# Routed half slots: the next rows' transposes go between the two parts of layer 1's transposes, and layer 2 multiplies high parts before low parts

## The reference, cut to what matters

```python
logits = x @ w_gate
noise_scale = np.log1p(np.exp(x @ w_noise))
noisy_logits = logits + noise_scale * noise
top2 = np.argpartition(-noisy_logits, 2, axis=1)[:, :2]
...
for e in range(E):
    for k in range(2):
        mask = top2[:, k] == e
        h = np.maximum(x[mask] @ w1[e], 0.0)
        out[mask] += top2_w[mask, k, None] * (h @ w2[e])
```

## Time and profile before

| | |
|---|---|
| median of 3 runs | 1065.53 us (1064.56 to 1066.09) |
| profiled execution, time | 1066.34 us |
| profiled execution, span first to last instruction | 1064.6 us |
| TensorE matmul, busy | 1001.9 us, 94% of the span |
| TensorE weight load, busy | 930.5 us, 87% |
| VectorE, busy | 748.9 us, 70% |
| ScalarE, busy | 475.4 us, 45% |
| GpSimd, busy | 165.6 us, 16% |
| mean granted TensorE clock | 0.964 of full speed |

### The profile page before, as it was taken

How to read it: one execution, slowest core, us unless ns; L and a number is a source line. 1 busy time by engine, 2 the same in 40 slices (tenths; PEclk the granted TensorE clock), 3 DMA queues, 4 the chain that set the end, 5 groups by cost and what they waited for, 6 DMA issues and landing times.

```text
span 1064.6 us, 25662 instructions
## 1 busy us (share of the span) xinstructions
PE 1001.9 (94%) x10317; PEld 930.5 (87%) x10317; DVE 748.9 (70%) x1812; ACT 475.4 (45%) x707; POOL 165.6 (16%) x164
## 2 busy tenths in 40 slices
PE   4777989999999999999999999999999999999995
PEld 4675878789889888889899999999999999999994
DVE  6989497389489488542548876767767786776774
ACT  4511423523532622422245554556465564654563
POOL 0000000021012012022305321122121112112111
PEclk7579899899999999999999999999999999999998
DMA  9160031042042033024575544335162425536221
GB/s 324 45 152 1 4 104 36 22 131 52 22 122 63 3 88 76 3 70 155 179 244 179 121 120 120 86 50 171 23 179 45 148 53 154 166 52 169 39 38 23
DMA packets 71459, 102.03 MB, mean 96 GB/s; under 512 B 28624, under 2 KB 59856, under 8 KB 70992
## 3 DMA queue, kind: packets, MB, share of 16 engines
q1 hardware_dynamic: 59296, 78.51, 24.4%
q0 software_dynamic: 10992, 20.70, 10.2%
q10 hardware_dynamic: 1088, 1.65, 0.5%
HBM read 140.53 MB, written 29.51 MB: 160 GB/s over the span
## 4 chain that ended last, share of the span: by engine, by line
PE 83%; DVE 7%; ACT 3%; issue 2%; SPq 2%; DMA 1%; DVEq 0%; POOLq 0%; ACTq 0%
PE ps L1595 39%; PE ps L1741 21%; PE ps L1636 7%; PE ps L1478 3%; PE ps L1572 2%; PE ps L1562 2%; PE ps L1552 2%; PE ps L1461 2%; PE ps L1652 1%; PE ps L1513 1%; PE ps L1523 1%; DVE prod L977 1%; DVE x L981 1%; DVE joint L1015 1%; PE ps L1534 1%
## 5 line engine op out<-in xcount | busy, mean ns | idle before, releaser
L1595 PE MATMUL ps<-xr,wr_in 128*128 128x512 f32 x972 | 240.0, 400 | 3.4 <-DVE xr L1045 1.9
L1741 PE MATMUL ps<-w2r,hbT 128*128 128x384 f32 x1320 | 237.0, 337 | 0.8 <-DVE hbT L1265 0.3
L1741 PEld LDWEIGHTS ps<-w2r,hbT 128*128 128x128 f32 x1320 | 227.9, 188 | 2.5 <-DVE hbT L1265 2.5
L1595 PEld LDWEIGHTS ps<-xr,wr_in 128*128 128x128 f32 x972 | 180.9, 190 | 44.3 <-DVE xr L1045 2.3
L1595 PE MATMUL ps<-xbT,w1r 128*128 128x256 f32 x1728 | 211.0, 283 | 0.0
L1595 PEld LDWEIGHTS ps<-xbT,w1r 128*128 128x128 f32 x1728 | 210.1, 192 | 0.0
L639 POOL DMA_INDIRECT out_rows<-yb,idx x55 | 91.1, 1656 | 380.0 <-DVE yb L1277 291.3
L1091 DVE TENSOR_TENSOR w1r<-w1s,w1r 128x768 fp32r<-128x768 f32 x128 | 121.2, 957 | 19.3 <-ACT w1r L776 17.1
L792 ACT ACTIVATE hbT<-ps 128x512 fp32r<-128x512 f32 x96 | 57.3, 597 | 170.5 <-PE ps L1595 169.0
L776 ACT CAST w1r<-w1s 128x768 fp32r<-128x768 f32 x128 | 104.4, 828 | 24.9 <-DMA w1s<-in_we 24.9
L1091 DVE TENSOR_TENSOR w2r<-w2s,w2r 128x768 fp32r<-128x768 f32 x128 | 113.8, 951 | 1.4 <-ACT w2r L780 1.4
(11 more groups left out here) (209 smaller groups left out, 1019.3 us busy)
## 6 DMA issues: line engine op xcount, KB each, us to landing
w1s<-in_we SPq DMA_DIRECT2D x32, 1536.0 KB
w2s<-in_we SPq DMA_DIRECT2D x32, 1536.0 KB
xb<-rows SPq DMA_DIRECT2D x25, 402.0 KB
kv_s<-in_kv SPq DMA_DIRECT2D x24, 384.0 KB, 3.3
k_s<-in_k SPq DMA_DIRECT2D x12, 512.0 KB, 3.6
joint<-in_q SPq DMA_DIRECT2D x24, 256.0 KB
out_rows<-padrow SPq DMA_DIRECT2D x13, 384.0 KB, 4.4
w_in<-in_w_blocks SPq DMA_DIRECT2D x3, 1152.0 KB, 10.6
```

Source lines behind the costliest of these rows:

```text
L1595: mm = pe.matmul(dst, w, m, start=(n == 0), stop=(n == len(todo) - 1))
L1741: mm = pe.matmul(ps[:, 6 + h, 0:MD], hbT[:, a, f, h * P:h * P + P], w2r[par][:, b, f], start=(f == 0 and n == 0), stop=(f == FT2 - 1 and n ...
```

## The change

In a half slot, `block_rows(j + 1)` is issued between `half_h(group, 0)` and `half_h(group, 1)` and no longer behind both. Layer 2 of a half slot becomes a function of its own: for each group of four f, first the eight matmuls with the high part of h, which wait for ScalarE's cast (`s_gh`), then the four with the low part, which wait for VectorE's subtraction (`s_g`). The matmuls are the same 24. There are four waits in place of two. Full slots keep their order.

```diff
-            def expert_out(j, par, half):
+            def expert_out(j, par):
-                for h in range(1 if half else 2):
+                for h in range(2):
...
-                        if half and f % 4 == 0:
-                            pe.wait_ge(s_g, j * 4 + (f // 2 + 2))
-                        elif not half and h == 0 and f % 2 == 0:
+                        if h == 0 and f % 2 == 0:
                             pe.wait_ge(s_g, j * 4 + (f // 2 + 1))
...
-                    mm.then_inc(p_yb, 2 if half else 1)
+                    mm.then_inc(p_yb, 1)
+
+            def half_expert_out(j, par):
+
+                for g in range(2):
+                    for a, low_parts in ((0, (0, 1)), (1, (0,))):
+                        pe.wait_ge(s_g if a else s_gh, j * 4 + (2 * g + 2))
+                        for f in range(4 * g, 4 * g + 4):
+                            for b in low_parts:
+                                mm = pe.matmul(ps[:, 6, 0:MD], hbT[:, a, f, 0:P], w2r[par][:, b, f],
+                                               start=(f == 0 and a == 0 and b == 0), stop=(f == FT2 - 1 and a == 1))
+                mm.then_inc(p_yb, 2)
...
                     half_h(group, 0)
+                    block_rows(j + 1, 1 - par, next_half)
                     half_h(group, 1)
...
-                block_rows(j + 1, 1 - par, next_half)
+                if not half:
+                    block_rows(j + 1, 1 - par, next_half)
...
-                expert_out(j, par, half)
+                if half:
+                    half_expert_out(j, par)
+                else:
+                    expert_out(j, par)
```

## The result

| | before | after |
|---|---|---|
| median of 12 runs each | 1065.81 us | 1062.60 us |
| range | 1063.70 to 1071.06 | 1060.48 to 1064.00 |
| profiled execution, time | 1066.34 us | 1063.64 us |
| span | 1064.6 us | 1061.9 us |
| mean granted TensorE clock | 0.964 | 0.964 |

The ratio is 0.9971 with a 95% interval of 0.9959 to 0.9982, so the change is faster by 0.29%. The forecast median was 1062.6 us.

A forecast was written before the change was run, and what follows sets the result against it. PE nearly always busy, VectorE's xbT chain limiting the gain: five slots of 0.71 - d - 0.05, one of 0.98 - d - 0.05, minus d at the end; with d = 0.19, 2.9 us off 1065.53 gives 1062.6 us, range 1061.0 to 1064.8.

The forecast's parts named there:

- The two waits and their size: Half slots: weight loads idle seven times for second hb (3.4 us) and for hbT's first low part (2.5 us).
- The six transposes fill the first wait; d = 0.19: Half slot: moved transposes fill the hb wait but delay the second four, and ScalarE's second cast, by d, 0.19 us.
- High parts first: Layer 2 of a half slot: loads start at 983.34 against 984.15, a head start of 0.81 us.
- Two more waits cost nothing: Layer 2 of a half slot: four waits in place of two, already satisfied, cost zero.
- What is late next: Next slot's first load: xbT late, a new wait of about 0.35 us, six times; gain 0.47 us, not 0.81.
- The end: Last half slot: TensorE's head start is worth nothing, the output's scaling comes the full delay, 0.19 us, later.
- The sum: Whole kernel: 4.23 - 7d over five slots, slot 6 and the end; 2.9 us gained with d = 0.19.
- A: Rival: VectorE's chain does not limit the next slot; about 4.7 us gained, 1060.8 us; chance 0.05.
- B: Rival: larger delay of the second transposes, 0.30 to 0.60 us; gain 2.1 to 0, say 1064.5 us; chance 0.24.
- C: Rival: late rows or slow transposes delay the second transposes; with d = 1.0, 2.8 us slower, 1068.3 us; chance 0.03.
- D: Rival: fourteen transposes in a row drop the clock to 1.2 GHz for layer 2; 22.6 us, 1088; chance 0.01.
- E: Rival: nothing changes, the gaps are the model's and the real array never idled; 1065.5 us; chance 0.04.

The follow-up runs named there:

- e5: The change, with quarter 2 of the next w1 put between the two hbT parts on ScalarE and VectorE; 1055.46 us, ratio 0.9961 to before.
- e3: The change, with the next rows' six transposes between the two parts issued twice; 1062.47 us, ratio 1.0020 to before.
- e1: Kernel before, with only the next rows' transposes moved between the two parts, layer 2 in old order; 1059.73 us, ratio 1.0000 to before.
- e2: Kernel before, with only layer 2's high parts first, the next rows' transposes still behind both parts; 1057.75 us, ratio 0.9976 to before.

## Why the prediction was right

**The two waits and their size.** Right: both are gone, 0.84 us in each half slot.

**The six transposes fill the first wait; d = 0.19.** Right: the second four end 1.09 us behind the first (1.10 forecast), and the second cast starts 981.36 - 980.18 = 1.18 us behind them, for 1.19; it was 1.00. Of the two bounds, 0.01 and 0.74, the step inside a running group was the one to take.

**High parts first; 0.81 us of head start.** Right: layer 2's loads begin 1.42 us behind the first transposes' start, against 2.24 before. The high part of part 0 is there at 980.85, ahead of them, and no wait of layer 2 is left.

**Two more waits cost nothing.** Right: 24 loads take 4.12 us, for 4.14.

**What is late next.** Right in kind: six waits of the next slot's first load behind `xbT`. One term was too small: TensorE answered 0.13 us behind the row's end of `xbT`, not 0.05, so the wait is 0.43 us, above the 0.3 to 0.4 that the prediction named as its sign. Why this answer takes longer than the 0.05 us read behind `hb` is not shown. Some of it comes back behind the wait, by the rows of slot 7, before in the first fence and after in the second:

```profile
681.02 0.68 PEld L1652 LDWEIGHTS ps<-ident,xb 128*128 128x128 f32 x6
```

```profile
671.87 8.70 PEld L1595 LDWEIGHTS ps<-xbT,w1r 128*128 128x128 f32 x72 [0.43 <-issue]
680.51 0.68 PEld L1652 LDWEIGHTS ps<-ident,xb 128*128 128x128 f32 x6
```

The 72 loads up to the next transposes take 680.51 - 671.87 = 8.64 us after, and 681.02 - 672.32 = 8.70 before. In half slot 26 it is 6.36 - 5.97 = 0.39 up to the load, and with some 0.06 behind it 0.45 for 0.47. That the answer's 0.08 us and these 0.06 nearly cancel is luck: the prediction had neither. Half slot 6 gives (672.32 - 665.70) - (671.87 - 665.90) = 0.65 and the same 0.06, 0.71 for the 0.74 forecast.

**The end.** Right: from the first transposes of slot 30 (before in the first fence, after in the second) to the last scaling it is 9.36 us (1042.31 to 1051.67), against 9.17 (1045.10 to 1054.27), 0.19 longer.

```profile
1045.10 0.60 PE L1726 MATMUL ps<-ident,hb 128*128 128x128 f32 x4
```

```profile
1042.31 0.60 PE L1726 MATMUL ps<-ident,hb 128*128 128x128 f32 x4
```

**The sum.** 2.9 us forecast. By the slots it is 5 x 0.45 + 0.71 - 0.19 = 2.77, and the stretch shows 2.80, the profiled times 2.70, the medians 3.2. That the median of after is the forecast 1062.6 us to the last digit is luck: the median of before moved from 1065.53 to 1065.81 us with more runs, and the ratio's interval is 2.5 us wide.

**The rivals.** A would have been right without VectorE's chain, which e5 shows: with that shortened, the slot gives 0.82. Its step, that the next slot could start, failed on the wait for `xbT`. B fell with d. C's slope is confirmed by e3, but its cause was absent: the list of waits has none of line 1652. D fell: the clock is 1.00 in the whole stretch, with fourteen transposes in a row. The Trainium skill, "TensorE: Matmul & The Clock Gate", Part 4: PE-mode transpose, says that transposes don't count as busy for the clock gate. The runs leave that open: neither fourteen transposes in a row nor the twenty of e3 (granted clock 1.00 from 560 to 1045 us) lowered the clock, and in both the pause between two products was shorter than before (in half slot 26 1.3 and 1.9 us, against 2.1). E fell: ratio 0.9971.

**What the prediction did not say** is how the gain divides. It worked the two parts into one sum; e1 and e2 show 0 for the move and 2.45 of the 2.80 for the order. With its own numbers this could have been read: 0.35 us to be won by the order alone without any d, and VectorE's slack of 0.71 left.

## What to carry to other kernels

Before removing a wait, write down the slack of each chain that meets the path again at the next join, and what the edit does to that slack; here the gain up to the next load was 0.71 - 0.19 - 0.13 = 0.39 us and not the 0.81 that the idle rows offered. An instruction slipped into an engine's gap still delays what other engines get from the instructions behind it, and in this kernel it cost seven times: 0.66 us more of it made the stretch 4.55 us longer (e3). Then look at what the last round does for a round that never comes: four unused w2 pieces held the end for 3.4 us.

## What the runs showed that I had not expected

The new wait of 0.43 us cost 0.06 us less than its length. Its matmul starts 0.01 us behind the load (985.56 and 985.55), where before it trailed by 0.18 us in the running stream (988.45 and 988.27), and the 72 loads take 8.64 us up to the next transposes and not 8.70. In e5 the slot that still waits has 8.63 us (666.11 to 674.74) and slot 11, which does not, 8.70 (728.40 to 737.10), so the difference goes with the wait. Why it is 0.06 and not 0.17 us is not shown. The view of waits names "issue" and not VectorE, so a new wait can look like no wait for anyone; the timeline tells.
